# Moving a weight-table load and a small bias computation between engines in a fused attention and expert kernel

## What is computed

```
bits   = (q @ proj > 0), (k @ proj > 0)          # proj: 64 x 6
scores = where(bucket(q) == bucket(k), q @ k.T / 8, -1e9)
x      = softmax(scores) @ v                     # 1536 x 512
logits = x @ w_gate + modality_bias[modality_id] # 1536 x 8
expert = argmax(logits)
out    = leaky((gate * relu(x_e @ w1) @ w2) @ w_in) @ w_out
```

## Time and profile before

| | |
|---|---|
| profiled execution, device time | 704.54 us |
| its span in the trace | 702.7 us |
| PE busy | 689.2 us (98%) |
| DVE busy | 467.9 us (67%) |
| ACT busy | 354.5 us (50%) |
| POOL busy | 235.3 us (33%) |
| mean granted clock of PE | 0.997 |

### The profile page before, as it was taken

How to read it: one execution, slowest core, us unless ns; L and a number is a source line. 1 busy time by engine, 2 the same in 40 slices (tenths; PEclk the granted TensorE clock), 3 DMA queues, 4 the chain that set the end, 5 groups by cost and what they waited for, 6 DMA issues and landing times.

```text
span 702.7 us, 12352 instructions
## 1 busy us (share of the span) xinstructions
PE 689.2 (98%) x4072; PEld 614.6 (87%) x4074; DVE 467.9 (67%) x1018; ACT 354.5 (50%) x694; POOL 235.3 (33%) x329
## 2 busy tenths in 40 slices
PE   7999999999999999999999999999999999999996
PEld 5899999999999998989998997888888888888885
DVE  5988989899999889514411225656676666766663
ACT  4888888888887892114411224333343333433331
POOL 7855465555558960512011245100016000010002
PEclk9999999999999999999999999999999999999999
DMA  6985866759373503961011129000003000010001
GB/s 168 219 252 151 212 199 157 213 123 259 81 177 90 195 27 134 292 212 41 34 60 47 57 84 321 1 0 0 0 20 101 0 0 0 6 55 0 0 1 60
DMA packets 48018, 71.09 MB, mean 101 GB/s; under 512 B 7326, under 2 KB 27502, under 8 KB 47974
## 3 DMA queue, kind: packets, MB, share of 16 engines
q1 hardware_dynamic: 40772, 55.93, 28.0%
q0 software_dynamic: 3472, 10.55, 4.8%
q10 hardware_dynamic: 3730, 4.07, 1.7%
HBM read 33.98 MB, written 17.30 MB: 73 GB/s over the span
## 4 chain that ended last, share of the span: by engine, by line
PE 87%; DVE 8%; ACT 2%; issue 1%; DMA 1%; ACTq 0%; POOLq 0%; POOL 0%; DVEq 0%
PE bank L995 7%; PE bank L1214 6%; PE bank L1204 6%; PE bank L1206 6%; PE bank L1205 6%; PE bank L1216 6%; PE bank L1215 6%; PE bank L1014 4%; PE bank L1016 4%; PE bank L979 4%; PE bank L980 4%; PE bank L1149 3%; PE bank L1153 3%; PE bank L1151 3%; PE bank L1121 3%; PE bank L1120 3%
## 5 line engine op out<-in xcount | busy, mean ns | idle before, releaser
L1321 ACT ACTIVATE probs<-bank,raffine 128x768 f32<-128x768 f32 x96 | 95.3, 993 | 29.3 <-DVE raffine L1598 29.0
L1590 DVE TENSOR_REDUCE bank<-bank 128x1 f32<-128x768 f32 x96 | 92.1, 960 | 4.7 <-PE bank L980 3.8
L845 POOL DMA_INDIRECT out<-o_sb,token_s x12 | 12.1, 1005 | 233.0 <-ACT o_sb L1513 154.6
L995 PE MATMUL bank<-cst,probs 128*128 128x128 f32 x576 | 80.4, 274 | 1.4 <-DVE pt_lo L1606 0.8
L1459 ACT ACTIVATE wi_hi<-ff_raw 128x512 fp32r (+1 forms) x48 | 30.4, 632 | 92.2 <-PE bank L1206 91.5
L995 PEld LDWEIGHTS bank<-cst,probs 128*128 128x128 f32 x576 | 67.8, 141 | 9.2 <-issue 4.3
L1899 DVE SCALAR_TENSOR_TENSOR ht_lo<-bank,ht_hi 128x512 fp32r<-128x512 f32 x28 | 19.0, 688 | 84.4 <-ACT ht_hi L1407 84.4
L1204 PE MATMUL bank<-x_hi,wi_hi 128*128 128x512 f32 (+1 forms) x192 | 74.3, 387 | 0.3 <-DVE x_lo L2014 0.3
L1606 DVE TENSOR_TENSOR pt_lo<-bank,pt_hi 128x384 fp32r<-128x384 f32 x128 | 70.3, 550 | 6.1 <-ACT pt_hi L1338 3.4
L1205 PE MATMUL bank<-x_lo,wi_hi 128*128 128x512 f32 (+1 forms) x192 | 73.9, 385 | 0.0
L1206 PE MATMUL bank<-x_hi,wi_lo 128*128 128x512 f32 (+1 forms) x192 | 73.9, 385 | 0.0
(11 more groups left out here) (315 smaller groups left out, 1692.2 us busy)
## 6 DMA issues: line engine op xcount, KB each, us to landing
stacks<-nat SPq DMA_DIRECT2D x84, 192.0 KB, 4.2
y_slots<-zeros SPq DMA_DIRECT2D x14, 512.0 KB, 5.5
w_raw<-in_moe_w SPq DMA_DIRECT2D x6, 1024.0 KB, 8.1
ff_raw<-in_moe_w_in SPq DMA_DIRECT2D x8, 512.0 KB, 9.0
ff_raw<-in_moe_w_out SPq DMA_DIRECT2D x4, 1024.0 KB, 10.9
y_slots<-y_sb ACTq DMA_DIRECT2D x14, 256.0 KB, 2.0
v_raw<-in_v SPq DMA_DIRECT2D x16, 192.0 KB, 3.6
x_rows<-x_out SPq DMA_DIRECT2D x8, 384.0 KB, 3.1
```

Of the source, the lines that this page charges most:

```text
L995: mm = pe.transpose(lane[1 + hf][:, t * P:t * P + P], probs[:, m % 3, kt * P:kt * P + P], C["ident"])
L1321: act.activation(probs[:, m % 3, :].rearrange("p (a c) -> p a c", a=2), s_ps[m % 2], ACT.Exp, bias=raffine[:, col, 1:2], scale=raffine[:, ...
```

## The change

It has three parts. The load of `proj` goes from ACT's queue to POOL's, as two DMAs of 64 partitions, and with the gate weights' four DMAs it now stands ahead of POOL's four clearings. The four copies that make `w_k` and `w_q` go from ACT to DVE. And `modality_bias` goes from POOL, at the head of its iteration n = 6, to DVE, behind all other work of its step 6.

```diff
 gpsimd
-            for par, rows in ((0, BOT), (1, TOP)):
-                for tile in (bq, bk):
-                    pool.memset(tile[rows, 1, par].bitcast(F32), 0.0).then_inc(feat_zeroed, 1)
+            for hf in range(2):
+                pool.dma_start(proj_raw[hf * HD:hf * HD + HD, :], proj).then_inc(proj_in, 16)
             for hf in range(2):
                 for par, at in ((0, 0), (1, HD)):
                     pool.dma_start(comb4[hf * HD:hf * HD + HD, :, par, at:at + E], ...)
+            for par, rows in ((0, BOT), (1, TOP)):
+                for tile in (bq, bk):
+                    pool.memset(tile[rows, 1, par].bitcast(F32), 0.0).then_inc(feat_zeroed, 1)
...
             for n in range(STEPS + QT + 2):
                 j, s = divmod(n, 2 * QT)
-                if n == QT:
-                    modality_bias()
 scalar
-            act.dma_start(proj_raw[:], proj.unsqueeze(0).broadcast_to([2, HD, BITS])).then_inc(proj_in, 16)
             act.dma_start(k_pair[:, :, 1, :], k_r[1]).then_inc(k_first, 16)
...
-            act.wait_ge(proj_in, 16)
-            act.wait_ge(w_zeroed, 4)
-            for w, apart in ((w_k, 2 * BITS), (w_q, BITS)):
-                for rows, at in ((TOP, HD), (BOT, 0)):
-                    act.activation(both_parts(w, rows, at, apart), twice(proj_raw, rows), ACT.Copy).then_inc(w_made, 1)
 vector
             dve.wait_ge(w_zeroed, 5)
+            dve.wait_ge(proj_in, 32)
+            for w, apart in ((w_k, 2 * BITS), (w_q, BITS)):
+                for rows, at in ((TOP, HD), (BOT, 0)):
+                    dve.tensor_copy(both_parts(w, rows, at, apart), twice(proj_raw, rows)).then_inc(w_made, 1)
...
+            def modality_bias():
+                dve.wait_ge(gate_in, 112)
+                then(dve.tensor_copy(mid_f[:], mid[:, :, 0]))
+                for b in range(2):
+                    dve.tensor_scalar(m01[:, b], mid_f[:], float(b), None, ALU.is_equal).then_inc(bias_step, 1)
+                dve.wait_ge(bias_step, 2)
+                for b in range(2):
+                    dve.tensor_tensor(bias2[:, b], tok(m01[:, b], E), row(mbias[:, b], TT), ALU.mult
+                                      ).then_inc(bias_step, 1)
+                dve.wait_ge(bias_step, 4)
+                dve.tensor_tensor(logits[:], bias2[:, 0], bias2[:, 1], ALU.add).then_inc(logits_set, 1)
...
                 step(n)
+                if n == QT:
+                    modality_bias()
```

## The result

The changed kernel takes 708.05 us (median of five runs, 707.90 to 708.54) against 704.54 before (here of five runs, 703.45 to 705.68): 1.0051 of its time, 95% interval 1.0036 to 1.0065. The forecast was 703.8 us, 0.7 faster; it became 3.5 us slower, outside the range of 702.2 to 705.7. The profiled execution took 708.4 us with a span of 706.6 us, 3.9 above the span before.

A forecast was written before the change was run, and what follows sets the result against it. Nothing is full before 13 us, DVE and POOL bind to 25.5, then PE with DVE close. Start -1.9 plus bias +1.2 gives -0.7 us: 704.54 to 703.8 us, range 702.2 to 705.7 for 8 in 10.

The forecast's parts named there:

- ACT's key load: Start: issued at 0.72 instead of 1.93, landing between 4.1 and 5.7; transposes at 5.6, a gain of 1.45 us.
- Rival B: Start: keys don't come earlier, through first-issue cost or bandwidth; gain 0.3 us, bias costs 1.2, 705.4 us; chance 0.13.
- POOL's new order: Start: six DMA issues plus clearing leave POOL free at 7.7; its ceiling lets step 0 start at 10.8, gain 2.15 us.
- The hash weights: DVE's copies and subtractions at the start: 1.4 us after proj lands at 4.6, sel_ready at 6.0, cost nothing.
- the cover is 0.75 us: Start: slack between sel_ready at 6.0 and DVE's first low part at 6.75.
- the start: Everything up to the first scores: step 0 at 11.05 instead of 12.95, gain 1.9 us, range 1.45 to 2.15.
- rival C: DVE's wait ahead of the first low part: proj lands late over POOL's queue; 705.7 us at landing 7.2; chance 0.15.
- The clock: PE's hash products: low clock starts step 0 at 11.5, high clock at 10.8; leaned to high, took 11.05.
- The bias: Six DVE instructions behind step 6: 1.3 us of DVE, PE waits 1.2 us in step 8, bounds 0 and 2.0.
- The 0.1 us of cover: Step 7's last low part ends at 32.64; PE, transposing, needs that bank at 32.73.
- the hold by POOL's subtraction: First bias instruction on DVE, beside POOL's subtraction for step 4: may lose 0 to 0.5 us, 0.2 taken.
- Rival A: Bias around step 8 is hidden because DVE may lag a step; only the start counts, 702.6 us; chance 0.17.

The follow-up runs named there:

- start alone: The changed kernel with the bias back on POOL, so only the start differs from the kernel before: 706.73 us, ratio 1.0039.
- the maximum: The changed kernel with DVE's four hash-weight copies written as the maximum of proj with itself, clearing still beside them: 704.33 us, ratio 1.0009.
- The filler: The changed kernel with twelve more zero matmuls on PE ahead of its wait for sel_ready: 705.98 us, ratio 1.0027.
- the bias alone: The kernel before with only modality_bias moved from POOL to DVE: 704.76 us, ratio 1.0014.
- the kernels with the clearing moved: The changed kernel with POOL's clearing between proj and gate DMAs: 704.81 us, ratio 1.0026; with the bias also back on POOL: 704.61 us, 1.0011.
- the kernel with the keys first: The kernel before with only ACT's key load issued ahead of proj: 701.94 us, ratio 0.9971; measured again, 702.00 us, 0.9980.

## Why the prediction was wrong

- **ACT's key load, right in kind.** It went out at 0.73 and landed at 4.9, both as forecast. The transposes started at 6.08 and not at 5.6, since the identity now landed last, at 6.0 against 4.3 before. The gain at that point was 1.0, not 1.45. Rival B falls with the landing.
- **POOL's new order, right.** Its clearing ended at 8.01 (forecast 7.7), and its key copy followed directly.
- **The hash weights: the step that failed.** The prediction has it as "DVE then does four copies at 0.17 and four subtractions at 0.17" and "Cost nothing; the cover is 0.75 us". proj landed at 6.0, not 4.6 (its second half 4.0 us after an issue at 1.98, where I took a gate DMA's 3.2 us from 1.4), and the copies took 2.7 us, not 0.7. `sel_ready` came at 9.54, forecast 6.0. With that the start, forecast as a gain of 1.9 us, became a loss of 2.7 (start alone). I had priced a copy by a subtraction; the maximum shows that a subtraction's price holds beside the clearing and a copy's doesn't. The Trainium skill, "SBUF — State Buffer", section "Who interferes with whom", lists copy, cast and tensor_scalar as what can, under conditions on their operands, exclude POOL, and says of two-input instructions that they meet only a POOL instruction that reads. The runs agree with both halves: 0.44 to 0.76 us for a copy beside the clearing, 0.18 for the maximum. The prediction used this section for the bias and for POOL's DMA issues, and not for these copies.
- **The evidence against rival C was misread.** I held that POOL's clearings ran beside DVE's without loss. Two clearings only show two clearings. Rival C had the right place (DVE's wait ahead of the first low part), but it let the landing be late and not the copies be long. On its own scale, on which the whole change is slower from 6.05 us on, the landing at 6.0 alone would have left the time where it was. Nor did its mechanism come true: POOL's first issue began 0.56 us late, at 1.27, and not 1.5 us late behind DVE's clearings, and the rest of the delay came behind the issue.
- **The clock: a term with the right two levels, of which the other came.** I leaned to a clock that stays up because PE idles less; the failed step made it idle 2.67 us in one piece, and the low clock lasted from about 9.5 to 16 us. The filler prices it at 1.7 us within the changed kernel. Of the 2.66 us by which step 7 is late, 1.36 are there when the hash products start; the other 1.30 come behind that, where the clock was low for longer than in the profile of the kernel before. How large that part is depends on the execution that one compares with: the same start ran at the low clock in the profile of the kernel before and at the high one in that of the bias alone. All six runs of the changed kernel have a mean clock of 0.992 to 0.996.
- **The bias, right and slightly low.** Forecast 1.3 us of DVE and 1.2 of PE, found 1.58 and 1.4 (1.0, between 0.2 and 1.8, by the ratio of the bias alone). The 0.1 us of cover and the hold by POOL's subtraction were as read, though for the copy, 0.63 us, it was longer than the 0.2 us taken. Rival A falls with PE's wait.
- **Together.** By the profiles 2.7 (start) and 1.4 (bias), less 0.2 later, make the 3.9 us.

What stays open: why the kernels with the clearing moved fall into two groups of runs by their clock, 2 to 3 us apart, when the kernel with the keys first never does in 18 runs; and why proj, over POOL's queue, landed 4.0 us after its issue.

## What to carry to other kernels

A price taken from one kind of instruction need not hold for another beside the same neighbour: before a small copy goes to DVE, look at what POOL does in that microsecond. Ahead of a point where PE waits, a delay can cost twice, once as such and once as a low clock behind it. And of a change in several parts each wants its own price: here one moved line gave 1.4 to 2.0 us, and the rest of the change cost more than that.

## Not expected of the hardware

- A DVE copy of 64x12 elements took 0.44 to 0.76 us beside POOL, each until an instruction of POOL ended (three times a clearing, once the key copy); with the clearing elsewhere 0.17 to 0.21 us (one of eight 0.32), and as a maximum beside the clearing 0.18.
- In the changed kernel POOL's DMAs of 1.5 KB landed 3.9 to 4.0 us after their issue, and its first issue of the kernel began at 1.27 us, where its first clearing had begun at 0.71.
- Taking one issue of 1.18 us away from ahead of the key load brought the landing from 6.93 to 4.9 in the changed kernel, 2.0 us and not 1.2. The load now travels in a stretch in which the DMA engines had stood at 0.63 of their share; that this is the reason is likely and not tested.
- The same program for the start ran with the granted clock at 0.50 from 8.6 to 12.0 us in one profile (the kernel before) and at 1.00 throughout in another (the bias alone), 0.9 us apart by step 7.
